# Four hand-written instruction orders changed in an attention, feed-forward and experts kernel on one core

## The chip, the cores and the metric

The kernel runs on one core of a Trainium2 chip. The core has a matrix engine (TensorE, "PE" in the profile, with its weight loads apart as "PEld"), VectorE ("DVE"), ScalarE ("ACT"), GpSimd ("POOL") and the queue that starts most transfers (SyncE, "SP"). Each engine works through its own list of instructions in order; between engines there are only semaphores. The metric is device time of one execution in microseconds (us), the median of some runs. Smaller is better.

## The reference, cut to what matters

Three layers follow one another, all in float32. The kernel computes them in one program.

```python
# 1. attention: q, k, v are (4, 8, 576, 64)
scores = scale * np.matmul(q, k.transpose(0, 1, 3, 2))
kth = np.partition(scores, -32, axis=-1)[..., -32:-31]      # the 32nd largest of each row
scores = np.where(scores >= kth, scores, -1000000000.0)
scores = scores - np.max(scores, axis=-1, keepdims=True)
attn = np.exp(scores)
attn = attn / (np.sum(attn, axis=-1, keepdims=True) + 1e-09)
out = np.matmul(attn, v)                                    # -> x, (2304, 512)
# 2. feed-forward, w_in (512, 2048), w_out (2048, 512)
h = x @ w_in
g = np.maximum(h, 0.0) + np.log1p(np.exp(-np.abs(h)))
x = g @ w_out
# 3. eight experts, w1 (8, 512, 1024), w2 (8, 1024, 512)
logits = x @ w_gate
expert_idx = np.argmax(logits, axis=1)
probs = softmax(logits)                                     # over the 8 experts
out[mask_e] = probs[idx, e][:, None] * (np.maximum(x[mask_e] @ w1[e], 0.0) @ w2[e])
```

## The kernel before, in words

**Blocks and steps.** Attention is cut into 72 blocks. A block is two score tiles of 128 rows by 576 keys. The loop `for i in range(-AHEAD, TAIL)` stands once in each engine's program, and step `i` of it works on several blocks at once: the scores of block `i + 1` (`scores`, L565, copied out by ACT in `scores_out`, L873 and L876), the 32 largest values of block `i` on DVE (`maxima` L1139 and `strike` L1145, four rounds of maxima and three of striking out), the mask and the exponentials of block `i - 1` (`cut_off` L884 on ACT, `mask` on POOL, `exponentials` L891 on ACT), and the product with v of block `i - 2` (`normalise` L897, `turn_probs` L579 and L582, `probs_out` L904, `times_v` L604).

**One block's way through the engines.** DVE finds the maxima. POOL turns them into biases (`biases`), ACT and POOL mask, ACT takes exponentials and sums them into `eps`. DVE turns the sum into `rden` (`reciprocals`, L1153 and L1156). ACT multiplies by it (`normalise`). PE then transposes the nine tiles of probabilities into PSUM (`turn_probs`), ACT copies them to `prT` (`probs_out`), and PE multiplies them with v (`times_v`). `turn_probs(i - 2)` stands behind `scores(i + 1)` on PE and waits until ACT has copied those scores; `probs_out(i - 2)` waits for the semaphore `transit_full`, which the last of the nine transposes raises.

**First stage, steps 0 to 9 (`i < MLP_AT`).** There is no feed-forward work yet. ACT and POOL split the feed-forward weights into a high and a low part in the same steps: `split_wo` (L941) with `low_wo` on POOL and a store by SP behind it, and `split_wi` (L947) with `low_wi`. Here DVE runs `reciprocals(n - 1)` at the end of block `n`. It waits there for `exponentials(n - 1)`, and the next block's maxima stand behind it.

**Second stage, steps 10 to 73.** PE adds one unit of the feed-forward layer to each step: `up` (L634 to L636) and `down` (L653 to L655). ACT and POOL compute the activation of the unit (`rectify`, `logarithm`, `h_high`, `softplus`, `h_low`). For blocks above 10, DVE runs `reciprocals(n - 2)` within block `n`, after the first round of striking out; POOL adds up the sum before it (`denominators`, L1502).

**Hand-over.** Behind the last feed-forward units stands an order written out by hand. The tokens of the last two tiles get their logits (`logits`, L676; copied by `logits_out`, L967). DVE picks the expert (`choose`, L1207 to L1215), PE counts the tokens of each expert (`count_late`, L699 and L700), DVE computes places and tables (`lanes`, `in_slots`, `slot_values`, L1375 to L1422), PE gathers the tables (`slots_late`, L706), and POOL fetches tokens by them. The first two expert tiles run between these steps: `turn_xs` (L716), `e_up` (L727 to L729), `e_relu_out` on ACT (L1010) and `relu` on DVE (L1318), one half of the rectified tile each, `turn_h` (L759), `e_h_out` (L1018) and `h_low` (L1331), `e_down` (L727 to L729). Then a loop over all expert tiles follows, which the change leaves as it is.

Of the kernel before, what the change touches and what calls it, by code (L numbers as in the profile page):

```python
# [20 lines left out]
def build(nc, q, k, v, w_in, w_out, w_gate, w1, w2, out):  # L21
# [15 lines left out]
    KE = EF // P  # L37
# [38 lines left out]
    MLP_AT = 2 * PAIRS + 2  # L76
# [29 lines left out]
    def wo_unit(i):  # L106
        return i - 1 if 0 <= i - 1 < UNITS else None
# [11 lines left out]
    with ExitStack() as ctx:  # L119
# [417 lines left out]
        def _(pe):  # L537
# [249 lines left out]
            for i in range(-AHEAD, TAIL):  # L787
                late = is_block(i - 2)
# [25 lines left out]
            for part in range(2):  # L814
# [26 lines left out]
                                 (1, 2): lambda: turn_tokens(LASTG, NT - 1, 4),  # L841
                                 (1, 3): lambda: logits(NT - 2, 3)}, halves=True, parts=(1,))
            logits(NT - 1, 7)
            turn_xs(1, 1)
            turn_h(0)
            e_up(1, rank_first, {(0, 1): count_late})
            e_down(0, 0, rank_first, {KE // 2: lambda: turn_h(1), KE // 2 + 1: slots_late}, halves=True)
            e_down(1, 1, rank_first, {KE - 2: lambda: turn_xs(2, 2)})
            pe.wait_ge(tiles_ready, 1)
            e_up(2)  # L850
# [15 lines left out]
        def _(act):  # L866
# [156 lines left out]
            for i in range(-AHEAD, TAIL):  # L1023
                now, late = is_block(i - 1), is_block(i - 2)
                if i < MLP_AT:
                    if late:
                        normalise(i - 2, 0)
                        normalise(i - 2, 1)
                    if is_block(i - 3):
                        x_out(i - 3)  # L1030
                    if now:
                        for t in cuts(i - 1):
                            cut_off(i - 1, t)
                    scores_out(i + AHEAD)
                    if wo_unit(i) is not None:
                        split_wo(wo_unit(i))
                    if now:
                        exponentials(i - 1, 0)
                        exponentials(i - 1, 1)
                    if late:  # L1040
                        probs_out(i - 2)
                    if wi_unit(i) is not None:
                        split_wi(wi_unit(i))
                    continue
# [60 lines left out]
            logits_out(NT - 2, 3)  # L1105
            logits_out(NT - 1, 7)

            e_relu_out(0)
            xs_out(1)
            gate_exps(1)  # L1110
            e_h_out(0, 0)
            e_relu_out(1)
            e_h_out(1, 1)
# [18 lines left out]
        def _(dve):  # L1132
# [29 lines left out]
            for n in range(BLOCKS):  # L1162
                for r in range(ROUNDS):
                    for t in range(2):
                        if r:
                            strike(n, t, r)
                    if r == 1 and n > MLP_AT:
                        reciprocals(n - 2)
                    for t in range(2):
                        maxima(n, t, r)  # L1170
# [195 lines left out]
            first_w2(0)  # L1366
            first_w2(1)

            relu(0)
            dve.wait_ge(logits_copied, NT)  # L1370
            choose(LAST, 1)
            xs_low(1)
            gates(LAST, 1)
            dve.wait_ge(counts_ready, 2)
            then(nc.vector.tensor_copy(new_count[:].rearrange("p t e -> p (t e)"),  # L1375
                                       psum[:, 7, 2 * E:4 * E]))
# [299 lines left out]
```

## Time and profile before

| what | us |
|---|---|
| median of 3 runs (lowest 1056.98, highest 1057.76) | 1057.62 |
| the profiled execution, its own time | 1057.62 |
| its span in the trace | 1055.4 |
| busy in the span: PE | 992.1 (94%) |
| busy: DVE | 817.1 (77%) |
| busy: ACT | 727.3 (69%) |
| busy: POOL | 711.8 (67%) |

The profiled execution took 1057.62 us, of which the span from the first to the last instruction is 1055.4; 2.2 us lie around it. The shares are averages over stages that differ much. The first stage ends near 109 us, attention with the feed-forward layer near 755 us, the hand-over near 840 us, and the expert tiles take the rest. The clock column of the windows is the share of its full speed (2.4 GHz) that TensorE was granted: 0.50 is 1.2 GHz. An idle time in brackets at a row's end tells how long the engine was idle before that row and who released it. Durations of rows overlap by a little, because an engine starts an instruction while the one before drains; the distance from one row's start to the next row's start is what an instruction costs its engine.

### The profile page before, as it was taken

The page shows a single profiled execution, that of the slowest core. Times are in us where ns is not written, and L with a number is a line of the kernel's source. Part 1 is how long each engine was busy: PE and PEld are TensorE (multiplying, and loading weights), DVE is VectorE, ACT ScalarE, POOL GpSimd, SP SyncE. Part 2 cuts the span into 40 slices and gives each one's busy share as a digit, 9 for nine tenths or more (in the row PEclk, how much of TensorE's full clock was granted, in tenths as well). Part 3 has the DMA queues.
Part 4 walks back from the last instruction along what each step waited for, and adds up shares of the span by engine and source line. Part 5 has one row for each costly group of instructions (what it writes and reads, how often), then busy time and mean ns, then how long its engine had stood idle before and what let it go on. Part 6 is the DMA issues. An engine that isn't in the chain of part 4 may idle for free.

```text
span 1055.4 us, 21464 instructions
## 1 busy us (share of the span) xinstructions
PE 992.1 (94%) x6878; PEld 806.1 (76%) x6879; DVE 817.1 (77%) x1744; ACT 727.3 (69%) x1390; POOL 711.8 (67%) x831
## 2 busy tenths in 40 slices
PE   3467899999999999999999999999999999999996
PEld 1344687788788788788788888888887788888875
DVE  7999999999999999999999999994345622222261
ACT  2888798889999998998988999998555111111140
POOL 2688899889899899899888899898351311111101
PEclk9855899999999999999999999999999999999999
DMA  9723225343335443323444332333481421111100
GB/s 316 252 90 130 102 93 206 126 145 120 110 113 182 140 159 120 115 107 120 157 154 148 123 120 100 121 120 120 143 328 69 165 95 52 40 40 40 40 20 20
DMA packets 43390, 130.98 MB, mean 124 GB/s; under 512 B 4320, under 2 KB 18656, under 8 KB 33056
## 3 DMA queue, kind: packets, MB, share of 16 engines
q1 hardware_dynamic: 40256, 120.09, 32.3%
q0 software_dynamic: 3040, 9.70, 2.7%
q8 instruction: 51, 0.84, 0.3%
q14 instruction: 43, 0.35, 0.1%
HBM read 111.95 MB, written 18.09 MB: 123 GB/s over the span
## 4 chain that ended last, share of the span: by engine, by line
PE 82%; DVE 7%; POOL 3%; ACT 3%; issue 2%; DMA 1%; SPq 1%; ACTq 0%; DVEq 0%; POOLq 0%
PE psum L604 9%; PE psum L565 8%; PE psum L634 7%; PE psum L727 6%; PE psum L729 6%; PE psum L728 6%; PE psum L653 6%; PE psum L636 6%; PE psum L635 6%; PE psum L655 6%; PE psum L654 6%; PE psum L579 5%; DVE top L1139 3%; DVE work L1145 2%; PE psum L759 2%
## 5 line engine op out<-in xcount | busy, mean ns | idle before, releaser
L1139 DVE MAX8 top<-work 128x8 f32<-128x576 f32 x432 | 305.5, 752 | 0.0
L1145 DVE MATCH_REPLACE8 work<-top,work 128x576 f32<-128x576 f32 x288 | 212.7, 750 | 0.0
L634 PE MATMUL psum<-x_parts,wi_hi 128*128 128x256 f32 x576 | 171.1, 297 | 0.0
L635 PE MATMUL psum<-x_parts,wi_hi 128*128 128x256 f32 x576 | 163.0, 283 | 0.0
L636 PE MATMUL psum<-x_parts,wi_lo 128*128 128x256 f32 x576 | 162.9, 283 | 0.0
L1514 POOL TENSOR_SCALAR pr<-sc,top 128x576 f32<-128x576 f32 x64 | 142.5, 2226 | 6.4
L604 PE MATMUL psum<-prT,vtok 128*64 128x128 f32 (+3 forms) x1600 | 117.1, 286 | 13.6 <-ACT prT L904 13.6
L604 PEld LDWEIGHTS psum<-prT,vtok 128*64 128x64 f32 (+1 forms) x1600 | 85.5, 144 | 52.7 <-issue 42.6
L565 PE MATMUL psum<-kT,qT 64*128 64x512 f32 (+3 forms) x640 | 112.8, 479 | 13.5 <-ACT sc L876 8.9
L1619 POOL DMA_INDIRECT out<-ys,dst_now x19 | 19.2, 1012 | 153.9 <-DVE ys L1341 151.9
L1510 POOL TENSOR_TENSOR pr<-sc,pr 128x576 f32<-128x576 f32 x80 | 114.2, 1432 | 9.2 <-ACT pr L884 9.2
L653 PE MATMUL psum<-wo_ring,h_hi 128*128 x288 | 119.1, 414 | 1.0 <-POOL h_lo L1528 0.9
L1522 POOL TENSOR_TENSOR hs<-hs,ab 128x512 f32<-128x512 f32 x72 | 93.6, 1300 | 34.3 <-ACT ab L927 33.9
L634 PEld LDWEIGHTS psum<-x_parts,wi_hi 128*128 128x128 f32 x576 | 109.9, 191 | 6.6 <-issue 2.0
L891 ACT ACTIVATE pr<-pr,bias 128x576 f32<-128x576 f32 x144 | 110.0, 766 | 4.9 <-POOL pr L1510 3.1
L655 PE MATMUL psum<-wo_ring,h_lo 128*128 x288 | 113.1, 393 | 0.0
L654 PE MATMUL psum<-wo_ring,h_hi 128*128 x288 | 112.7, 391 | 0.0
L565 PEld LDWEIGHTS psum<-kT,qT 64*128 64x128 f32 (+1 forms) x640 | 57.4, 195 | 70.0 <-issue 64.4
L635 PEld LDWEIGHTS psum<-x_parts,wi_hi 128*128 128x128 f32 x576 | 110.2, 191 | 0.2
L636 PEld LDWEIGHTS psum<-x_parts,wi_lo 128*128 128x128 f32 x576 | 110.2, 191 | 0.0
L897 ACT ACTIVATE pr<-pr,rden 128x576 f32<-128x576 f32 x144 | 104.4, 784 | 6.4 <-DVE rden L1156 6.4
L1139 DVE MAX8 top<-sc 128x8 f32<-128x576 f32 x144 | 101.6, 751 | 7.7 <-ACT sc L876 7.7
(206 smaller groups left out, 2235.1 us busy)
## 6 DMA issues: line engine op xcount, KB each, us to landing
wo_ring<-wo_parts SPq DMA_DIRECT2D x72, 1024.0 KB, 4.8
wo_parts<-wo_ring SPq DMA_DIRECT2D x8, 1024.0 KB, 3.9
kT<-in_k SPq DMA_DIRECT2D x16, 288.0 KB, 3.6
qT<-in_q SPq DMA_DIRECT2D x16, 288.0 KB, 4.4
vtok<-in_v SPq DMA_DIRECT2D x16, 256.0 KB, 2.8
wo_raw<-in_moe_w_out SPq DMA_DIRECT2D x1, 4096.0 KB, 14.1
wi_raw<-in_moe_w_in SPq DMA_DIRECT2D x4, 1024.0 KB, 14.6
x_rows<-x2tok SPq DMA_DIRECT2D x16, 256.0 KB, 2.5
```

The costliest lines, as they stand in the source:

```text
L565: mm = nc.tensor.matmul(to[rows, :], qT[h * HD:(h + 1) * HD, p, cols], kT[h * HD:(h + 1) * HD, p, keys], start=True, stop=True)
L604: mm = nc.tensor.matmul(x_raw_at[h * HD:(h + 1) * HD, cols], vtok[rows, p, c, h * HD:(h + 1) * HD], probs, start=(c == 0), stop=(c == FULL))
L634: nc.tensor.matmul(ps[:, part, :], wi_hi[:, u, kk, f], hi, start=first, stop=False)
L635: nc.tensor.matmul(ps[:, part, :], wi_hi[:, u, kk, f], lo, start=False, stop=False)
L636: mm = nc.tensor.matmul(ps[:, part, :], wi_lo[:, u, kk, f], hi, start=False, stop=last)
L653: nc.tensor.matmul(psum[:, 6 + a, :], high, hi, start=(f == 0), stop=False)
L654: nc.tensor.matmul(psum[:, 6 + a, :], high, lo, start=False, stop=False)
L655: mm = nc.tensor.matmul(psum[:, 6 + a, :], low, hi, start=False, stop=(f == KF - 1))
L1139: nc.vector.max(top[:, at, 8 * r:8 * r + 8], sc[:, at, :] if r == 0 else work[:, t, :]).then_inc(topk_step, 1)
L1145: nc.vector.match_replace(work[:, t, :], top[:, at, 8 * r - 8:8 * r], sc[:, at, :] if r == 1 else work[:, t, :], TAKEN).then_inc(topk_step, 1)
L1510: nc.gpsimd.tensor_tensor(to, sc[:, at, :], to, ALU.subtract).then_inc(masked, 1)
L1514: nc.gpsimd.tensor_scalar(to, sc[:, at, :], top[:, at, TOPK - 1:TOPK], OUT, ALU.is_lt, ALU.mult).then_inc(mask_step, 1)
```

## The change

No instruction is added or removed. Four orders change.

1. ACT, steps 2 to 9: `probs_out(i - 2)` moves from behind `split_wo` and the two `exponentials` to a place right behind `scores_out(i + 1)`.
2. DVE, second stage: `reciprocals(n - 2)` moves from the round `r == 1` to the round `r == 2` of block `n`, for n above 10.
3. PE, hand-over: `count_late` moves ahead of `turn_xs(1, 1)` and `turn_h(0)`, out of `e_up(1)`. `slots_late` moves from ahead of product 5 of `e_down(0)` to ahead of its product 3, and so ahead of `turn_h(1)`, which stays ahead of product 4.
4. ACT and DVE, hand-over: ACT runs `gate_exps(1)` ahead of `e_relu_out(0)`. DVE runs `choose(LAST, 1)` ahead of `relu(0)` and `gates(LAST, 1)` ahead of `xs_low(1)`.

```diff
             logits(NT - 1, 7)
+            count_late()
             turn_xs(1, 1)
             turn_h(0)
-            e_up(1, rank_first, {(0, 1): count_late})
-            e_down(0, 0, rank_first, {KE // 2: lambda: turn_h(1), KE // 2 + 1: slots_late}, halves=True)
+            e_up(1, rank_first)
+            e_down(0, 0, rank_first, {KE // 2 - 1: slots_late, KE // 2: lambda: turn_h(1)}, halves=True)
...
                     scores_out(i + AHEAD)
+                    if late:
+                        probs_out(i - 2)
                     if wo_unit(i) is not None:
                         split_wo(wo_unit(i))
                     if now:
                         exponentials(i - 1, 0)
                         exponentials(i - 1, 1)
-                    if late:
-                        probs_out(i - 2)
                     if wi_unit(i) is not None:
                         split_wi(wi_unit(i))
...
+            gate_exps(1)
             e_relu_out(0)
             xs_out(1)
-            gate_exps(1)
...
-                    if r == 1 and n > MLP_AT:
+                    if r == 2 and n > MLP_AT:
                         reciprocals(n - 2)
...
-            relu(0)
             dve.wait_ge(logits_copied, NT)
             choose(LAST, 1)
+            relu(0)
+            gates(LAST, 1)
             xs_low(1)
-            gates(LAST, 1)
             dve.wait_ge(counts_ready, 2)
```

**ACT, one step of the first stage.** Before, the score copies are followed by the cast of the second weights, the exponentials, and then the copy to `prT`:

```order
L873 ACTIVATE sc<-psum 128x128
L876 ACTIVATE sc<-psum 128x512 x2
L941 CAST wo_ring<-wo_raw 128x1024
L891 ACTIVATE pr,eps<-pr,bias 128x576 x2
L904 COPY prT<-psum 128x1152
L947 CAST wi_hi<-wi_raw 128x1024
L897 ACTIVATE pr<-pr,rden 128x576 x2
```

The same place in the changed program, where every line number is one higher:

```order
L874 ACTIVATE sc<-psum 128x128
L877 ACTIVATE sc<-psum 128x512 x2
L905 COPY prT<-psum 128x1152
L942 CAST wo_ring<-wo_raw 128x1024
L892 ACTIVATE pr,eps<-pr,bias 128x576 x2
L948 CAST wi_hi<-wi_raw 128x1024
L898 ACTIVATE pr<-pr,rden 128x576 x2
```

The copy out of PSUM now stands ahead of the cast and the exponentials.

**DVE, one block of the second stage.** Before, the reciprocal follows the first striking out:

```order
L1139 MAX top<-sc 128x8 x2
L1145 MATCH_REPLACE work<-top,sc 128x576 x2
L1156 RECIPROCAL rden<-den 128x2
L1139 MAX top<-work 128x8 x2
L1145 MATCH_REPLACE work<-top,work 128x576 x2
```

In the changed program it follows the second:

```order
L1140 MAX top<-sc 128x8 x2
L1146 MATCH_REPLACE work<-top,sc 128x576 x2
L1140 MAX top<-work 128x8 x2
L1146 MATCH_REPLACE work<-top,work 128x576 x2
L1157 RECIPROCAL rden<-den 128x2
```

Two maxima and two strikings now come ahead of the reciprocal that did not.

**PE, the hand-over.** Before, behind the last logits come the transposes of tokens and of `hr`, and the counts stand behind the first products of `e_up(1)`:

```order
L676 MATMUL psum<-wg,x2T 128x8 x4
L716 MATMUL psum<-ident,xs 128x128 x4
L759 MATMUL psum<-ident,hr 128x128 x8
L736 REGISTER_ALU
L727 MATMUL psum<-w_hi,xsT_hi 128x512
L728 MATMUL psum<-wbuf,xsT_hi 128x512
L729 MATMUL psum<-w_hi,xsT_lo 128x512
L699 MATMUL psum<-onehot,tri 128x16
L700 MATMUL psum<-onehot,ones 128x16
```

In the changed program:

```order
L676 MATMUL psum<-wg,x2T 128x8 x4
L699 MATMUL psum<-onehot,tri 128x16
L700 MATMUL psum<-onehot,ones 128x16
L716 MATMUL psum<-ident,xs 128x128 x4
L759 MATMUL psum<-ident,hr 128x128 x8
L736 REGISTER_ALU
L727 MATMUL psum<-w_hi,xsT_hi 128x512
```

The two counting products have moved ahead of twelve transposes.

## Rows read from the trace of the kernel before

**Rows 1.** Windows: start:end, length, busy of PE, PEld, DVE, ACT, POOL, clock, DMA, GB/s.

```profile
60.00:80.00 20.00, 14.38 (x76) 9.68 (x74) 19.93 (x47) 17.61 (x32) 17.20 (x17) 0.50 0.26 105
...
440.00:460.00 20.00, 20.00 (x158) 16.59 (x157) 19.46 (x43) 18.59 (x38) 18.65 (x21) 1.00 0.43 152
```

**Rows 2.** ACT timeline, step 3: start, duration, operation, count, idle before.

```profile
38.60 1.04 ACT L947 CAST wi_hi<-wi_raw 128x1024 fp32r<-128x1024 f32 x1 [2.13 <-DMA wi_raw<-in_moe_w_in]
39.55 1.44 ACT L897 ACTIVATE pr<-pr,rden 128x576 f32<-128x576 f32 x2
...
43.49 1.05 ACT L941 CAST wo_ring<-wo_raw 128x1024 fp32r<-128x1024 f32 x1
...
48.90 0.78 ACT L897 ACTIVATE pr<-pr,rden 128x576 f32<-128x576 f32 x1 [0.88 <-DVE rden L1156]
```

**Rows 3.** ACT timeline, one whole step (step 7) of the first stage.

```profile
78.58 1.44 ACT L897 ACTIVATE pr<-pr,rden 128x576 f32<-128x576 f32 x2 [0.97 <-DVE rden L1156]
...
82.82 1.06 ACT L941 CAST wo_ring<-wo_raw 128x1024 fp32r<-128x1024 f32 x1
83.75 0.80 ACT L891 ACTIVATE pr<-pr,bias 128x576 f32<-128x576 f32 x1
...
85.39 1.12 ACT L904 COPY prT<-psum 128x1152 f32<-128x1152 f32 x1
86.41 1.05 ACT L947 CAST wi_hi<-wi_raw 128x1024 fp32r<-128x1024 f32 x1
88.48 0.78 ACT L897 ACTIVATE pr<-pr,rden 128x576 f32<-128x576 f32 x1 [1.02 <-DVE rden L1156]
```

**Rows 4.** PE timeline, the transposes of probabilities in that step.

```profile
83.20 1.94 PE L579 MATMUL psum<-ident,pr 128*128 128x128 f32 x8 [1.56 <-ACT sc L876]
84.93 0.42 PE L582 MATMUL psum<-ident,pr 128*128 128x128 f32 x1
```

**Rows 5.** DVE timeline, the sum at the end of that step's block.

```profile
88.10 0.14 DVE L1153 TENSOR_REDUCE den<-eps 128x2 f32<-128x4 f32 x1
```

**Rows 6.** PE timeline, the same transposes at the other clock.

```profile
133.92 1.06 PE L579 MATMUL psum<-ident,pr 128*128 128x128 f32 x8
134.82 0.27 PE L582 MATMUL psum<-ident,pr 128*128 128x128 f32 x1
```

**Rows 7.** ACT and PE timelines, step 9, the last of the first stage.

```profile
98.37 1.44 ACT L897 ACTIVATE pr<-pr,rden 128x576 f32<-128x576 f32 x2 [1.03 <-DVE rden L1156]
...
105.68 1.10 ACT L904 COPY prT<-psum 128x1152 f32<-128x1152 f32 x1
...
106.83 0.48 PE L604 MATMUL psum<-prT,vtok 128*64 128x128 f32 x2 [1.75 <-ACT prT L904]
```

**Rows 8.** Waits of the whole run: who for whom, us in total, times, longest.

```profile
DVE rden L1156 <- POOL den L1502: 24.1, 27, 8.6
...
ACT pr L897 <- DVE rden L1156: 6.4, 7, 1.1
```

**Rows 9.** DVE, ACT and PE timelines, the beginning of the second stage.

```profile
121.64 0.17 DVE L1156 RECIPROCAL rden<-den 128x2 f32<-128x2 f32 x1 [1.00 <-POOL den L1502]
...
124.48 1.41 DVE L1139 MAX8 top<-work 128x8 f32<-128x576 f32 x2
...
150.74 0.17 DVE L1156 RECIPROCAL rden<-den 128x2 f32<-128x2 f32 x1
...
151.69 0.79 ACT L897 ACTIVATE pr<-pr,rden 128x576 f32<-128x576 f32 x1
...
152.84 0.38 PE L579 MATMUL psum<-ident,pr 128*128 128x128 f32 x2
```

**Rows 10.** PE and DVE timelines, the hand-over to the experts.

```profile
809.59 0.33 PE L759 MATMUL psum<-ident,hr 128*128 128x128 f32 x1 [0.27 <-ACT hr L1010]
...
809.89 0.18 DVE L1213 TENSOR_TENSOR onehot<-r_eq,tidx 128x16 f32<-128x16 f32 x1
...
821.11 0.41 PE L759 MATMUL psum<-ident,hr 128*128 128x128 f32 x2 [0.89 <-DVE hr L1318]
```

## The prediction, made before the changed kernel was run

> **What bounds the kernel now.** I read the windows first, because the shares of the page average over unlike stages. They show two regimes [rows 1]. In the first stage DVE is busy 19.93 of 20 us and TensorE 14.38, at a granted clock of 0.50 (its level of 1.2 GHz). In the second stage TensorE is busy 20.00 of 20 at clock 1.00 (2.4 GHz), with DVE at 19.46 close behind. So in the first stage time is lost by whatever makes a block's step longer than DVE's own, and in the second by whatever holds up TensorE.
>
> Then I read one step of the first stage on the ACT timeline [rows 3]. From one multiplication by rden (78.58) to the next (88.48) it is 9.90 us, and ACT waited only 1.02 us of that, for DVE. DVE starts the sum that ACT waits for at 88.10, and its row shows no wait [rows 5]: DVE came straight from its maxima. The page's list of waits says the same: ACT waits for rden 7 times, 6.4 us in all [rows 8]. ACT is nearly as full as DVE here, and its order fits closely: while PE transposes from 83.20 to 84.93 + 0.42 = 85.35 [rows 4], ACT does the weight cast (82.82) and the exponentials (83.75), and reaches the copy to prT at 85.39, when the transposes have just ended.
>
> **Edit 1, the copy to prT ahead of cast and exponentials.** The copy still needs the end of the transposes, and these still need the score copies. So ACT now stands idle from 82.82 until 85.39, which is 2.57 us, with nothing to do. Behind it in its list are the weight cast (POOL's low part and SP's store wait for it), the exponentials (DVE's sum and its next block wait for them) and the next multiplication. The new step on ACT, from rows: from the multiplication to the end of the score copies 43.49 - 39.55 = 3.94 [rows 2], wait 2.57, copy to prT 86.41 - 85.39 = 1.02, cast 83.75 - 82.82 = 0.93, exponentials 85.39 - 83.75 = 1.64 [rows 3], second cast 39.55 - 38.60 = 0.95 [rows 2]. The sum is 11.05 us against 9.90, so 1.15 us more per step, and ACT takes DVE's place as the bound.
>
> How many steps: steps 4 to 8 are whole, 5 x 1.15 = 5.75. In step 2 ACT waited 2.13 us for the load of the weights [rows 2], and the new wait falls almost wholly into that; I take 0.2. Step 3 had its transposes at the higher clock, where nine of them take 134.82 + 0.27 - 133.92 = 1.17 [rows 6] instead of 2.15. The wait is then about 1.6 and the step 3.94 + 1.6 + 4.54 = 10.1, against 48.90 - 39.55 = 9.35 [rows 2]: 0.75. Step 9 therefore begins 0.2 + 0.75 + 5.75 = 6.7 us late. In step 9 the copy to prT came 105.68 - 98.37 = 7.31 us after the multiplication, held by exponentials that wait for masks [rows 7]. Now it goes ahead of them: 3.94, less about 0.7 because this step cuts off one tile and not two (an estimate: half of the 1.44 that a pair of this shape takes in [rows 3]), plus 2.57, is 5.8. That gives 1.5 back. The product with v that opens the dense work of TensorE (106.83 [rows 7]) starts 6.7 - 1.5 = 5.2 us late, and from there on TensorE has no gaps to make it up. **Term 1: +5.2 us.** Bounds of the wait, which the trace does not show in this place: 1.6 with transposes at clock 1.00 and 2.57 at 0.50. I take the second, since [rows 1] has the whole stage at 0.50.
>
> A rule speaks against this term. The Trainium skill, "Perfetto Trace Analysis", section "Identifying the Most-Contended Engine", ranks engines by occupancy, though for TensorE it prefers other measures. Read over the whole span it would leave a stall on ACT (69% busy) unpriced, and the time would stay at 1057.6. The trace disagrees for this stage: there DVE has 19.93 of 20 and ACT 17.61.
>
> **Edit 2, the reciprocal one round later.** It moves past one round of maxima and striking. From the reciprocal at 121.64 to the next round of maxima at 124.48 it is 2.84 us [rows 9], of which such a round takes some 2.78 and the reciprocal the rest (an estimate). Waiting behind the reciprocal are ACT's multiplication and PE's transposes. In the middle of the stage this is covered. There DVE waits for POOL's sum again and again (27 waits, 24.1 us, of which 8.6 and 2.9 come after its last block [rows 8]), so DVE will run up to 2.78 us ahead, and the reciprocal again comes right after the sum. At the beginning it isn't covered, since DVE arrives late from the first stage. Step 8 now begins at 88.48 + 0.2 + 0.75 + 4 x 1.15 = 94.03, and its exponentials end 3.94 + 2.57 + 1.02 + 0.93 + 1.64 = 10.10 later, at 104.13. DVE's sum follows at 104.2 instead of 88.10 + 9.90 = 98.0 [rows 3, 5], so DVE is 6.2 us late. In step 14 the reciprocal stood at 150.74 [rows 9]. It moves by 6.2, by 2.78 for the round, and by -1.09 for the wait before 121.64 that goes with its restart [rows 9]: 7.9. With 0.2 to release ACT it allows the multiplication at 158.84. Without edit 2 that would be at 151.69 + 5.2 = 156.89 [rows 9]. The transposes need the first half of it, 0.92 later, so 159.76, against 152.84 + 5.2 = 158.04 [rows 9]. **Term 2: +1.7 us.** A DVE block takes (150.74 - 121.64) / 3 = 9.70 us here [rows 9], and TensorE's steps are longer on the mean, or DVE would not wait 25 times. So some steps later the lag is gone, but TensorE keeps what it lost. Bounds: 0, if ACT's slack before the transposes is larger than it looks, and 2.8, the whole round.
>
> **Edits 3 and 4, the hand-over.** The choice of experts is ready at 809.89 + 0.18 = 810.07 [rows 10]. The counts now stand ahead of the transposes of hr on PE, and both halves of hr are now made after DVE's choice and ACT's gate exponentials. So these transposes move from 809.59 to about 811.0, 1.4 us later. The tokens' low parts wait behind DVE's five gate operations (about 0.2 us each, an estimate by the 0.18 of [rows 10]), and e_up(1) starts some 1.5 us late, less the counts that have left it. But what ends last is DVE's chain from the counts to the tables. It began behind gates and low parts before and does so now, at the same time. PE waited for it 0.89 us before the transposes at 821.11 [rows 10]. PE now comes later and waits less, and slots_late fills the place of the 0.89. Bounds: -0.9 (that wait gone and nothing added) and +1.6 (nothing absorbed). I take 0, since the chain on DVE is as long as before. The tables come a little earlier for POOL's gathers, which nobody waits for. **Term 3: 0.**
>
> **Sum.** 5.2 + 1.7 + 0 = +6.9 us on a span of 1055.4, so 1062.3. The profiled execution had 2.2 us around its span and took 1057.62, which is also the median of the runs. Forecast: **1064.5 us**.
>
> **The rivals.**
> *The clock decides for less.* If TensorE is granted 1.00 through the first stage, the wait is 1.6 and a step 10.1, only 0.2 above 9.90. Step 9 begins 0.2 + 0.75 + 1.0 = 2.0 late and gives back 2.4, so PE is at -0.4. DVE is at +1.5, and the late reciprocal then costs 2.6. Sum +2.2: 1059.8. For it: step 3 had the higher clock. Against: TensorE has even less to do per us than in [rows 1]. The Trainium skill, "TensorE: Matmul & The Clock Gate", section "What's actually happening", says that activity releases the throttle. By that rule a thinner stage stays at 0.50, and the trace agrees so far as its busy stretch has 1.00 and its thin one 0.50.
> *Nothing is lost.* The transposes' end is modelled. If their semaphore came well before 85.35, ACT would wait little, and its 1.02 us of slack would take it. Then 1057.6. Against: the same transposes at the other clock take 1.17 [rows 6], about half of the 2.15, so the model follows the clock.
> *Faster.* DVE's 12.6 us of waits inside the second stage (24.1 - 8.6 - 2.9) [rows 8] are what edit 2 frees. If DVE, and not TensorE, paced that stage, they would come back: 5.2 - 12.6 = -7.4, so 1050.2. It decides from the point at which ACT's multiplications there are released by DVE. Against: the 7 waits of ACT for rden [rows 8] are those of the first stage, as at 48.90, 78.58, 88.48 and 98.37 [rows 2, 3, 7], and TensorE shows 20.00 of 20 [rows 1].
> *Worse.* The late reciprocal also delays ACT's exponentials, POOL's sum and so the next reciprocal. If this ring can't run at 9.7 us, the lag of term 2 grows by a few tenths per step through the seven steps until 200 us: +3 more, 1067.5.
>
> **How the numbers follow.** Chances: forecast 0.70 (its own range, with both bounds of terms 2 and 3 at once, is +4.3 to +9.6, so 1061.9 to 1067.2), clock 0.12, nothing lost 0.06, faster 0.05, worse 0.07. A difference under 0.2%, 2.1 us, can't be told from none, so "same" is 1055.5 to 1059.7. The clock case lies at that edge and is shared out: faster 0.05, same 0.10, slower 0.85. The range reaches from the clock case to the worse case: 1059.5 to 1067.5.
>
> **What would show it.** Term 1: in steps 4 to 8, ACT's copy to prT is idle before for about 2.5 us with TensorE as releaser, DVE's sum waits for ACT by about 1 us, a step takes 11.05, and the clock stays 0.50 past 113 us. Term 2: ACT's multiplications of steps 11 to 16 wait for rden, by up to 2 us, and none after 210 us; the waits of DVE for the sum shrink. Term 3: a wait of about 1.4 us before the counts, none at the second transposes of hr, and the expert loop entered at the old time plus 6.9. I am wrong if steps 4 to 8 keep 9.9 us, or if TensorE shows waits inside the second stage that take back its lag.

## The result and the profile after

| | before | after |
|---|---|---|
| median of the runs | 1057.62 us (5 runs, 1056.98 to 1058.06) | 1065.46 us (5 runs, 1063.24 to 1068.03) |
| profiled execution | 1057.62 us, span 1055.4 | 1067.26 us, span 1065.0 |

The medians differ by 7.8 us, where +6.9 (1064.5) was forecast. The ratio, which takes in four more runs of the changed kernel, is 1.0078, with a 95% interval of 1.0063 to 1.0092, or +6.7 to +9.7 us. The changed kernel also scatters more: its five runs lie within 4.8 us, where the kernel before has 1.1 here and 1.5 to 2.0 in the larger batches below. Its profiled execution lies at the slow end, so the trace below shows more loss (+9.6) than the median has.

Where the loss arises is read from the starts of a few instructions that both kernels have. The table gives, in us, the place in before, and how much later it is in the profiled execution of each kernel. T(n) are TensorE's transposes of block n; the column before the last is the third turn of hr, after which the experts' loop runs at the old pace.

| profiled execution | product with v that opens the dense work | T(8) | T(9) | T(10) | T(71) | third turn of hr | whole |
|---|---|---|---|---|---|---|---|
| before | 106.83 | 115.79 | 124.28 | 133.92 | 738.21 | 839.94 | 1057.62 |
| after | +3.98 | +3.23 | +5.87 | +8.52 | +8.47 | +9.61 | +9.64 |
| edit 1 alone | +2.35 | +1.54 | +1.55 | +1.50 | +2.17 | +2.31 | +2.36 |
| edit 2 alone | -0.10 | -1.29 | +0.03 | +0.10 | +0.90 | +1.05 | +1.12 |
| edits 3, 4 alone | +0.31 | -0.32 | -0.31 | -0.33 | -0.35 | +0.09 | +0.15 |
| edits 2, 3, 4 | -0.38 | -1.13 | -0.23 | -0.17 | +0.63 | +1.89 | +1.93 |

Three places carry the loss of the changed kernel: the first stage, the step from block 8 to block 10, and the hand-over. Its lag does not grow in the 600 us between T(10) and T(71).

Small differences in the first columns are no effects. The kernel before and those with edit 2 alone, edit 3 alone, edits 3 and 4 (with and without fill) and edits 2, 3 and 4 have the same instructions up to there. Their product with v lies between 106.45 and 107.24 and their T(8) between 114.50 and 115.79, and before, from which all lags are counted, has the latest T(8) of the six.

**The first stage.** One step of ACT in the changed kernel, the answer to [rows 3] (line numbers are one higher now):

```profile
83.01 1.44 ACT L898 ACTIVATE pr<-pr,rden 128x576 f32<-128x576 f32 x2
...
89.51 1.12 ACT L905 COPY prT<-psum 128x1152 f32<-128x1152 f32 x1 [2.44 <-PE psum L582]
90.53 1.05 ACT L942 CAST wo_ring<-wo_raw 128x1024 fp32r<-128x1024 f32 x1
91.47 0.78 ACT L892 ACTIVATE pr<-pr,bias 128x576 f32<-128x576 f32 x1
...
93.00 1.03 ACT L948 CAST wi_hi<-wi_raw 128x1024 fp32r<-128x1024 f32 x1
93.94 1.44 ACT L898 ACTIVATE pr<-pr,rden 128x576 f32<-128x576 f32 x2
```

The copy to prT waits 2.44 us for the transposes and everything else of the step stands behind it. From one multiplication to the next it is 93.94 - 83.01 = 10.93 us, where [rows 3] have 9.90. DVE's sum, which had no wait in [rows 5], now has one:

```profile
93.13 0.16 DVE L1154 TENSOR_REDUCE den<-eps 128x2 f32<-128x4 f32 x1 [0.93 <-ACT pr L892]
```

The step before this one is shorter, 83.01 - 72.94 = 10.07:

```profile
72.94 1.44 ACT L898 ACTIVATE pr<-pr,rden 128x576 f32<-128x576 f32 x2
...
78.58 1.12 ACT L905 COPY prT<-psum 128x1152 f32<-128x1152 f32 x1 [1.58 <-PE psum L582]
```

The same copy waited 1.58 us only. The windows say why: start and end, length, busy time of PE, PEld, DVE, ACT and POOL, then the clock. (The clock column needs care at the start of a trace. In before it shows 1.00 up to about 44 us, though the eight transposes at 33.07 take 1.97 us, as at clock 0.50. Below, only later windows are used, and the transposes' durations beside them: 1.94 us for eight at 0.50, 1.06 at 1.00.)

```profile
60.00:80.00 20.00, 12.39 (x68) 7.97 (x66) 18.06 (x42) 15.97 (x30) 15.74 (x16) 0.59 0.26 105
44.50:75.00 30.50, 21.20 (x111) 14.51 (x111) 27.59 (x63) 23.45 (x41) 23.76 (x23) 0.50 0.21 87
75.20:78.40 3.20, 1.14 (x9) 0.97 (x9) 3.20 (x8) 1.80 (x5) 3.03 (x4) 0.96 0.32 131
78.60:95.50 16.90, 11.88 (x65) 7.82 (x65) 15.82 (x37) 14.46 (x26) 13.91 (x13) 0.51 0.20 81
```

In the stretch of [rows 1] DVE fell from 19.93 to 18.06 of 20 us and TensorE from 14.38 to 12.39. The clock isn't 0.50 all through the stage, it goes up to 1.00 for short stretches, and transposes that fall into one are over in about half the time: at 77.26 eight of them take 1.08 us, in the next step, at 87.32, 1.94.

**Blocks 8 to 10.** The page's list of waits, the answer to [rows 8] (who for whom: us, times, longest):

```profile
DVE rden L1157 <- POOL den L1503: 26.8, 27, 8.6
...
ACT prT L905 <- PE psum L582: 18.2, 9, 2.4
...
DVE den L1154 <- ACT pr L892: 6.4, 7, 2.0
...
ACT pr L898 <- DVE rden L1157: 2.9, 2, 2.5
```

The copy to prT is new in the list with 18.2 us in 9 waits. ACT's waits for the reciprocal went from 7 to 2, and one of them has 2.51 of the 2.9 us. It is here, in ACT's, DVE's and TensorE's own rows, where [rows 9] had no such wait:

```profile
128.37 0.75 DVE L1146 MATCH_REPLACE8 work<-top,work 128x576 f32<-128x576 f32 x1
129.03 0.16 DVE L1157 RECIPROCAL rden<-den 128x2 f32<-128x2 f32 x1
```

```profile
129.23 1.44 ACT L898 ACTIVATE pr<-pr,rden 128x576 f32<-128x576 f32 x2 [2.51 <-DVE rden L1157]
```

```profile
130.15 1.73 PE L579 MATMUL psum<-ident,pr 128*128 128x128 f32 x7 [2.82 <-ACT pr L898]
```

The reciprocal of block 9 comes at 129.03, behind the striking of the round it was moved past. ACT's multiplication had waited 2.51 us for it and TensorE's transposes 2.82 us for ACT. Then come these windows:

```profile
123.00:129.60 6.60, 4.32 (x34) 3.58 (x32) 6.60 (x15) 4.09 (x11) 6.04 (x9) 0.98 0.00 0
129.80:136.50 6.70, 6.35 (x20) 5.46 (x21) 6.70 (x15) 5.96 (x12) 4.06 (x5) 0.52 0.00 0
```

Behind the wait TensorE has the clock 0.50 for a whole stretch of dense work, 6.35 of 6.7 us busy. By 136.7 it is at 1.00 again. In before the clock is 1.00 without a break from 113.3 to 1050 us. From T(9) to T(10) it is 12.29 us against 9.64, so this stretch cost 2.65 us more. It is a loss of this execution. That every run of the changed kernel has it isn't shown, and the medians leave little room for it: edit 1 alone (+4.6) and edits 2, 3 and 4 (+2.7) already add to 7.3 of the 7.8 us.

**The hand-over**, the answer to [rows 10]:

```profile
818.65 0.44 PE L699 MATMUL psum<-onehot,tri 128*128 128x16 f32 x2 [1.29 <-DVE onehot L1214]
818.92 0.59 PE L700 MATMUL psum<-onehot,ones 128*128 128x16 f32 x2
819.35 1.09 PE L716 MATMUL psum<-ident,xs 128*128 128x128 f32 x4
820.24 1.92 PE L759 MATMUL psum<-ident,hr 128*128 128x128 f32 x8
```

```profile
819.30:822.50 3.20, 3.04 (x14) 2.67 (x15) 1.71 (x10) 1.60 (x4) 0.00 (x0) 0.53 0.01 3
```

The counts wait 1.29 us for DVE's choice, and behind this wait too the clock is 0.50 for over 3 us, so that the 8 transposes of hr take 1.92 us instead of the 1.04 that they take in the experiments below at clock 1.00.

What holds TensorE at the end of the hand-over is DVE's chain from the counts to the tables. In before it starts at 812.30, as soon as the counts are there:

```profile
812.30 0.17 DVE L1375 COPY new_count<-psum 128x16 f32<-128x16 f32 x1 [0.62 <-PE psum L700]
```

In the changed kernel the counts come early, but the tokens' low part ahead of the chain waits for ACT's `xsT_hi`, which waits for the transposes of tokens, and these stand behind the counts now:

```profile
821.52 0.69 DVE L1324 TENSOR_TENSOR xsT_lo<-psum,xsT_hi 128x512 fp32r<-128x512 f32 x1 [1.32 <-ACT xsT_hi L1004]
822.13 0.17 DVE L1376 COPY new_count<-psum 128x16 f32<-128x16 f32 x1
```

The choice is 8.53 us later than before (818.42 against 809.89), the start of the chain 9.83. So the chain starts 1.30 us late, and it ends as late: `lanehot` is written at 829.66 instead of 819.84, and TensorE's tables (L706) start at 830.13, at the moment it is done.

### The profile page after: what moved, and what is told of

Read it like the earlier page. It is cut to its first block, busy times and chain, and to the rows that moved or that the text cites. A ratio compares the mean times of both kernels' runs of the same rounds, so it can differ in the third digit from the quotient of the medians.

```text
span 1065.0 us, 21464 instructions
## 1 busy us (share of the span) xinstructions
PE 994.3 (93%) x6878; PEld 809.2 (76%) x6879; DVE 817.9 (77%) x1744; ACT 726.6 (68%) x1390; POOL 712.0 (67%) x831
## 4 chain that ended last, share of the span: by engine, by line
PE 83%; ACT 6%; DVE 3%; issue 3%; POOL 2%; DMA 1%; SPq 1%; ACTq 0%; DVEq 0%; POOLq 0%
PE psum L604 8%; PE psum L565 7%; PE psum L634 7%; PE psum L579 7%; PE psum L727 6%; PE psum L729 6%; PE psum L728 6%; PE psum L653 6%; PE psum L636 6%; PE psum L635 6%; PE psum L655 6%; PE psum L654 6%; PE psum L759 2%; PE psum L676 1%; DMA wo_raw<-in_moe_w_out 1%
## 5 line engine op out<-in xcount | busy, mean ns | idle before, releaser
L579 PE MATMUL psum<-ident,pr 128*128 128x128 f32 x576 | 83.0, 289 | 32.8 <-ACT sc L877 28.9
```

The source lines that it names most:

```text
L579: mm = nc.tensor.transpose(transit[:, j // 3, j % 3 * P:(j % 3 + 1) * P], pr_of(n)[:, first_key(t) + c * P:first_key(t) + (c + 1) * P], id ...
```

## The experiments

Twelve kernels, each timed beside the kernel before on the same chip. Differences below are of medians of one batch; the interval is that of the ratio, which need not be the ratio of the medians. One unit in the third decimal of a ratio is 1.06 us.

| kernel | median | before | ratio, 95% interval |
|---|---|---|---|
| edit 1 alone | 1062.02 | 1057.42 | 1.0041 (1.0027 to 1.0054) |
| edit 2 alone | 1058.76 | 1057.42 | 1.0013 (1.0004 to 1.0022) |
| edits 3 and 4 alone | 1058.40 | 1057.42 | 1.0010 (1.0001 to 1.0019) |
| edits 2, 3 and 4 | 1060.07 | 1057.42 | 1.0027 (1.0016 to 1.0038) |
| copy between cast and exponentials | 1056.75 | 1057.48 | 0.9993 (0.9984 to 1.0002) |
| copy early in step 9 alone | 1056.72 | 1057.48 | 0.9996 (0.9987 to 1.0005) |
| after, first six reciprocals as before | 1064.52 | 1057.48 | 1.0062 (1.0048 to 1.0076) |
| after, filled first stage | 1063.69 | 1057.48 | 1.0056 (1.0042 to 1.0070) |
| edits 3 and 4, filled wait | 1057.86 | 1057.63 | 1.0003 (0.9994 to 1.0012) |
| edit 3 alone | 1058.21 | 1057.63 | 1.0006 (0.9997 to 1.0015) |
| before, filled first stage | 1056.74 | 1057.63 | 0.9992 (0.9983 to 1.0001) |
| copy between in steps 2 to 8, early in 9 | 1057.06 | 1057.63 | 0.9995 (0.9986 to 1.0004) |

### The edits one by one

**Edit 1 alone.**

```diff
+                    if late:
+                        probs_out(i - 2)
                     if wo_unit(i) is not None:
...
-                    if late:
-                        probs_out(i - 2)
```

> The kernel before with edit 1 alone: the copy to prT ahead of cast and exponentials in the first stage. Theory A (ACT's wait for the transposes costs time in every step there): the copy waits about 2.5 us in steps 4 to 8, the product with v that opens the dense work starts 4 to 5 us late (106.83 before), and TensorE keeps that to the end without losing more at the start of the second stage, because the reciprocal still stands behind the first round. So +4 to +5: 1062. Rival B (the time is lost by the late reciprocal and the hand-over, and the first stage only shifts waits about): within 1.5 us of the kernel before.

Measured: +4.6 us by the medians. Theory A holds, rival B falls. In its trace the product with v comes 2.35 us late (theory A had 4 to 5), ACT's copy waits as in the changed kernel, and the transposes of block 9 have only the short wait:

```profile
87.78 1.12 ACT L904 COPY prT<-psum 128x1152 f32<-128x1152 f32 x1 [2.45 <-PE psum L582]
```

```profile
125.83 0.63 PE L579 MATMUL psum<-ident,pr 128*128 128x128 f32 x4 [0.20 <-ACT pr L897]
```

Its five runs lie between 1059.98 and 1062.76, the profiled one being the lowest. In its step 5 eight transposes take 1.17 us and the step 10.16, in its step 7 they take 1.94 and the step 10.93, which shows what a run can win. Steps 4 to 6 are all of the short kind (10.20, 10.16 and 10.08).

**Edit 2 alone.**

```diff
-                    if r == 1 and n > MLP_AT:
+                    if r == 2 and n > MLP_AT:
```

> The kernel before with edit 2 alone: the reciprocal one round later. Theory A: DVE isn't late from the first stage, so the 2.78 us of a round, less the 1.09 us wait that goes, leave the reciprocals of the first blocks of the second stage about 1.7 us later, and ACT's slack takes most of it: 0 to +1, so 1058. Rival B: the late reciprocal costs by itself what the changed kernel lost at the start of the second stage, +2.8 or more (1060.5 and above). Rival C: DVE's waits of 12.6 us inside the stage come back as time, below 1055.

Measured: +1.3 us, between A and B. Rival C falls: DVE's waits for POOL's sum are 25.3 us in 25 times, where before has 24.1 in 27, and no time came back. ACT's multiplications of four blocks wait:

```profile
123.39 1.44 ACT L897 ACTIVATE pr<-pr,rden 128x576 f32<-128x576 f32 x2 [1.20 <-DVE rden L1156]
...
133.09 1.44 ACT L897 ACTIVATE pr<-pr,rden 128x576 f32<-128x576 f32 x2 [0.76 <-DVE rden L1156]
...
152.50 0.78 ACT L897 ACTIVATE pr<-pr,rden 128x576 f32<-128x576 f32 x1 [0.76 <-DVE rden L1156]
```

These steps are 9.70 us apart, which is DVE's block, where TensorE alone needs 9.46. From T(9) to T(13) TensorE loses 0.07, 0.24, 0.24 and 0.20 us, and none from T(13) to T(14). That POOL's sum, and not DVE's place in its list, holds the reciprocal again from there is an inference. In this execution T(8) happened to be 1.29 us early, and the wait of 1.51 us at T(9) took that back: here DVE sets T(9).

**Edits 3 and 4 alone.** The diff is that of the change for these two.

> The kernel before with edits 3 and 4 alone, the hand-over to the experts. Theory A (from the changed kernel's trace, where the lag grew from 8.5 to 9.6 us over the hand-over): about +1.1, half of it a wait of TensorE before the counts and half a stretch at clock 0.50 behind it: 1058.7. Rival B (the prediction's own term 3): 0, the wait of 0.89 us that goes pays for it.

Measured: +1.0 us. In its profiled execution, which was a quick one (1057.77), the wait for the choice is there but the clock stays 1.00:

```profile
809.79 0.40 PE L699 MATMUL psum<-onehot,tri 128*128 128x16 f32 x2 [1.29 <-DVE onehot L1214]
...
810.73 1.04 PE L759 MATMUL psum<-ident,hr 128*128 128x128 f32 x8
...
820.57 2.22 PE L706 MATMUL psum<-inslot,lanehot 128*128 128x108 f32 x18
```

```profile
808.00:823.00 15.00, 12.70 (x74) 10.65 (x74) 12.64 (x46) 3.03 (x7) 0.00 (x0) 1.00 0.01 2
```

DVE's chain is late here too, by less:

```profile
811.97 0.69 DVE L1324 TENSOR_TENSOR xsT_lo<-psum,xsT_hi 128x512 fp32r<-128x512 f32 x1 [0.63 <-ACT xsT_hi L1004]
812.58 0.16 DVE L1376 COPY new_count<-psum 128x16 f32<-128x16 f32 x1
```

The choice is 0.33 us earlier than in before and the chain 0.28 later, so it starts 0.61 us late. From T(71) to the third turn of hr TensorE loses 0.44 us here, against 1.14 in the changed kernel and 1.26 in the kernel with edits 2, 3 and 4, which both have the stretch at 0.50 and a chain that starts 1.30 late. Its runs form two groups: seven from 1057.19 to 1058.42 and three from 1060.02 to 1060.40. One more took 3296 us, an outlier that no median feels. The stretch at 0.50 costs some 0.7 us in those two traces (1.14 against 0.44), less than the 2.4 us between the groups. But it can be longer. The changed kernel with a filled first stage, described below, has the same hand-over; there it lasts twice as long, and the hand-over loses 2.19 us:

```profile
816.60:823.40 6.80, 6.37 (x23) 5.47 (x24) 4.75 (x24) 2.46 (x5) 0.00 (x0) 0.52 0.00 1
```

That such a stretch makes the group at 1060 fits, but no execution of it was profiled.

**Edits 2, 3 and 4.**

> The changed kernel with edit 1 undone, so edits 2, 3 and 4. Theory A: the sum of edit 2 alone (0 to +1) and the hand-over (+1.1), so 1058.7 to 1059.7, and no wait of TensorE of 2.8 us at the transposes of block 9, since DVE isn't late. Rival B (edit 2 costs the same whatever the first stage does): +1.1 and +4, 1062.5 or more.

Measured: +2.7 us (1060.07, 0.4 above theory A's range), where edit 2 alone (1.3) and the hand-over (1.0) add to 2.3. So edit 2 costs about 1.5 us where DVE comes in time, and rival B falls. The wait at block 9 is 1.07 us, and the clock stays 1.00 behind it. With edit 1 alone (4.6) this makes 7.3 us of the 7.8. Whether the rest is an interaction can't be told from differences that are each uncertain by about 1 us.

### How much of the wait must be filled

**The copy between cast and exponentials** (the kernel before, with a half of edit 1).

```diff
                     if wo_unit(i) is not None:
                         split_wo(wo_unit(i))
+                    if late:
+                        probs_out(i - 2)
                     if now:
...
-                    if late:
-                        probs_out(i - 2)
```

> The kernel before with a half of edit 1: the copy to prT stands behind the weight cast and ahead of the exponentials. Theory A (a step costs what ACT's idle wait adds beyond its 1.02 us of slack): the cast fills 0.93 of the wait, so the copy waits about 1.6 us, the step is 10.1 at clock 0.50 (+0.2), step 9 begins 1 to 2 us late and gives 1.5 back: total -0.5 to +0.7, near 1057.5. Rival B (what costs is that the exponentials come behind the copy, and so DVE's sum, whatever ACT's wait): +3 or more.

Measured: -0.7 us, just below theory A's range and, by the interval, no sure gain. The copy waits still, but the cast has taken 0.93 of it, and a step is 10.0 (69.66 - 59.67 = 9.99):

```profile
59.67 1.44 ACT L897 ACTIVATE pr<-pr,rden 128x576 f32<-128x576 f32 x2
...
63.61 1.05 ACT L941 CAST wo_ring<-wo_raw 128x1024 fp32r<-128x1024 f32 x1
66.18 1.12 ACT L904 COPY prT<-psum 128x1152 f32<-128x1152 f32 x1 [1.51 <-PE psum L582]
...
69.66 1.44 ACT L897 ACTIVATE pr<-pr,rden 128x576 f32<-128x576 f32 x2
```

A wait of 1.51 us costs 0.09 us per step, one of 2.44 costs 1.03: it is the part beyond ACT's slack that counts. The slack is not the 1.02 us of [rows 3] alone. ACT's work in a step is 11.05 - 2.57 = 8.48 us by the prediction's own rows, so that of the 9.90 it has 1.42 to spare. A part of the rest is a second wait in the step of [rows 3], for the scores:

```profile
81.69 0.28 ACT L873 ACTIVATE sc<-psum 128x128 f32<-128x128 f32 x1 [0.18 <-PE psum L565]
```

With 8.48 both steps come out: 8.48 + 1.51 = 9.99 and 8.48 + 2.44 = 10.92. Rival B falls, since the exponentials stand behind the copy here too.

**The copy early in step 9 alone.**

```diff
+                    if late and i == MLP_AT - 1:
+                        probs_out(i - 2)
                     if wo_unit(i) is not None:
```

> The kernel before with edit 1 in step 9 alone, the last of the first stage, where the exponentials wait for masks. Theory A: no step is longer, and the product with v comes 1.5 us earlier (105.3 instead of 106.83); TensorE keeps this through the second stage: -1 to -1.5, 1056.2. Rival B: block 9's reciprocal (121.64) or DVE holds TensorE there, and the gain is waited off: 0.

Measured: -0.8 us (-0.4 by the ratio), short of theory A's range and by the interval no sure gain. The product with v comes 1.22 us earlier, at 105.61, and T(71) is 1.02 earlier:

```profile
105.61 0.91 PE L604 MATMUL psum<-prT,vtok 128*64 128x128 f32 x6 [1.21 <-ACT prT L904]
```

In this trace the gain that the prediction gave to step 9 (1.5 us) is there, with 1.22: the product is 0.84 us earlier than in any of the six executions with the old first stage.

**Both places at once.** The copy between cast and exponentials in steps 2 to 8, ahead of both in step 9.

> The kernel before with the copy to prT between the cast and the exponentials in steps 2 to 8, and ahead of both in step 9; nothing else. Theory A: each of the two alone gave -0.7 to -0.8 because step 9's copy comes earlier, and that gain is one and the same: -0.5 to -1.5, 1056.5. Rival B (the gains add): -1.5 or more, 1056.0 or less.

Measured: -0.6 us, as theory A has it; -1.5, where rival B begins, lies at the edge of the interval. No kernel here is surely faster than before.

### The late reciprocal and the clock

**After, with the first six late reciprocals in their old place.**

```diff
-                    if r == 2 and n > MLP_AT:
+                    if r == (1 if n < MLP_AT + 7 else 2) and n > MLP_AT:
```

> The changed kernel with the reciprocals of the first six blocks of the second stage back in their old place, all later ones a round later. Theory A (edit 2 costs only at the start of that stage, where DVE is late, and is covered by POOL's sum in the rest): no wait of TensorE before the transposes of block 9 and no clock of 0.50 behind it, so edit 1 alone (+4.4) and the hand-over (+1.0): 1062.8, against 1065.5 of the changed kernel. Rival B (the late reciprocals cost a little in every block): within 1 us of the changed kernel.

Measured: +7.0 us, 1.7 more than theory A gave and 0.8 less than the changed kernel, so the medians decide nothing. The trace does: the opening product is 5.62 us late, T(9) 5.54 and T(10) 5.49, with no wait for the reciprocal and the clock at 1.00. The loss between blocks 8 and 10 is gone. But the first reciprocal that is late makes ACT wait at block 15, and TensorE is 0.65 us later from there:

```profile
188.37 0.78 ACT L898 ACTIVATE pr<-pr,rden 128x576 f32<-128x576 f32 x1 [1.08 <-DVE rden L1157]
```

So theory A was too narrow: here a late reciprocal costs something at block 15 too. The reading is that DVE hadn't yet got ahead of TensorE there; no run tests it. From there to T(71) the lag stays, 6.14 at T(16) and 6.25.

**After, with the first stage of TensorE filled.** In the two waits of each step TensorE transposes the identity, 9 and 4 times.

```diff
+                if late and i < MLP_AT:
+                    filler(9)
                 if late:
                     turn_probs(i - 2)
+                if late and i < MLP_AT:
+                    filler(4)
```

> The changed kernel with 9 and 4 more transposes of the identity per step in the first stage, in the places where TensorE waits, into a bank that nobody reads there. Theory A (ACT waits for the transposes' duration, and this hangs on the clock): if the fuller stage is granted 1.00, the wait falls from 2.5 to 1.6 us, a step to 10.1, and the time by 3 us or more, to 1062 or less. Rival B (the clock has no part in it): no difference to the changed kernel, or slower by the work added.

Measured: +6.2 us, 1.6 less than the changed kernel and about half of what theory A gave; the two intervals overlap. The mean clock of the stage rose from 0.57 to 0.84, not to 1.00:

```profile
57.00:105.00 48.00, 31.27 (x175) 20.86 (x175) 44.39 (x99) 38.86 (x68) 39.24 (x36) 0.57 0.21 88
```

```profile
57.00:105.00 48.00, 31.78 (x244) 24.18 (x242) 45.02 (x101) 39.68 (x69) 39.42 (x36) 0.84 0.22 88
```

The other executions of this first stage without the fill, edit 1 alone and the one with six reciprocals back, have 0.62 and 0.61. But the transposes that ACT waits for gained nothing: in steps 3 to 9 four of seven still take 1.94 us, as in the changed kernel, and ACT's copies of these steps wait 14.9 us in all, against 15.2 there, 13.8 with edit 1 alone and 16.8 with the six reciprocals back. The product with v is 3.89 us late, against 3.98. So this trace, the slowest of its five runs, does not show the mechanism of theory A; whether the fill saves time stays open. Behind a wait of 3.16 us at block 9 the clock fell here too, as in the changed kernel.

**Before, with the same fill** (6 and 4).

> The kernel before with 6 and 4 more transposes of the identity per step in the first stage, in TensorE's waits. Theory A (DVE bounds that stage, so a higher clock of TensorE is worth nothing there): more of the stage at clock 1.00, steps still 9.90, 1057 to 1057.5. Rival B (the first stage of the kernel before also loses time by the clock): 1056 or less.

Measured: -0.9 us, between the two, and by the interval no sure gain. The steps stay 9.90 us with the mean clock of 57 to 105 us at 0.82 instead of 0.50, as theory A has it: there DVE is the bound. T(8) comes 0.75 us earlier, with clock 0.84 instead of 0.63 in the opening of the dense work, 105 to 116 us. But unfilled executions of the same first stage have T(8) up to 1.29 us earlier, so this isn't shown to be the fill's doing.

**Edits 3 and 4 with the wait filled**, 10 transposes of the identity ahead of the counts.

```diff
+            for _ in range(10):
+                nc.tensor.transpose(psum[:, 4, 0:P], ident[:], ident[:])
             count_late()
```

> Edits 3 and 4 alone, as before, with 10 transposes of the identity ahead of the late counts, where TensorE waits 1.3 us, into a bank that nobody reads there. Theory A (the hand-over costs nothing by its waits, and what it costs comes from executions in which the wait is followed by a stretch at clock 0.50): 1057.5, no loss, and no execution near 1060. Rival B (the delayed transposes of hr cost by themselves): 1058.4 as without the fill, or more.

Measured: +0.2 us, and none of 11 runs above 1058.86, where three of the ten (without the outlier) were at 1060 without the fill. That none is near 1060 fits theory A, but three in ten against none in eleven is thin. Against it, the trace with the wait filled loses the same 0.44 us in the hand-over, and DVE's chain again starts 0.61 us late: the wait before the counts is filled (no idle is left before them), so it isn't that wait which costs the 0.44. Rival B's +0.8 lies within the interval.

**Edit 3 alone.**

> The kernel before with edit 3 alone, the counts and the late slots earlier on TensorE, with the order of DVE and ACT as it was. Theory A: the wait before the counts is the same 1.3 us (it is for DVE's choice), so it has the whole cost of the hand-over: 1058 to 1058.5. Rival B (the later relu and gates of edit 4 carry it): 1057.5.

Measured: +0.6 us, one run of 11 at 1060.33. The wait before the counts is the same 1.29. The hand-over loses 1.11 us in the trace, more than edits 3 and 4 together, and at the same clock of 1.00. The late slots now wait:

```profile
820.67 2.22 PE L706 MATMUL psum<-inslot,lanehot 128*128 128x108 f32 x18 [0.79 <-DVE lanehot L1242]
```

They wait for DVE's chain, which starts 1.25 us late here (at 812.67, with the choice at 809.01): DVE waits 1.79 us for `xsT_hi` and does the five gate operations after it. With edit 4 the gate operations fill that wait, and the chain is 0.61 late. So edit 4 pays for a part of edit 3. In six of the seven traces with edit 3 the loss of the hand-over follows the chain: 0.61 late and 0.44 to 0.46 lost three times, 1.25 to 1.30 late and 1.11 to 1.26 lost three times. The seventh is the one with the long stretch at 0.50: its chain is 1.48 late, and TensorE, itself behind, loses 2.19.

## Why the prediction was right

The time and the main mechanism came out as forecast; the sizes of the steps within term 1, the way in which term 2 arose and the reason given for term 3 did not.

- **Bound of the first stage and edit 1's wait: right.** Forecast 2.57 us idle and a step of 11.05; measured 2.44 and 10.93. The step with transposes at clock 1.00, forecast as 10.1, was 10.07. The half edit confirms that ACT's slack stands between cost and none. The slack is 1.42 us, as the prediction's sum of 11.05 implies, and not the 1.02 that its text names.
- **Term 1, +5.2: near by the medians, for partly wrong reasons.** Edit 1 alone measured +4.6 (interval +2.9 to +5.7), and the product with v was 2.35, 3.98 and 5.62 us late in three traces of the same code. In the changed kernel's trace steps 4 to 8 cost 3.95 us where 5.75 were forecast, because two of the five took 10.07 and 10.56: the reading of [rows 1], a window of 20 us, as a clock of 0.50 for the whole stage was wrong. Step 3 cost 1.58 instead of 0.75. The prediction took its fast transposes for a property of the step, but in the changed kernel they take 1.94. Step 9 gave back 2.15 instead of 1.5. The stage began 0.44 late for no cause that is known. So the rival "the clock decides for less" was half true: not a rival but a part of every execution.
- **Term 2, +1.7: near for edit 2 alone (+1.3), too small in the changed kernel's trace.** DVE's part was forecast well: its reciprocal of block 9 moved by 7.4 us, where 7.9 was worked out. (That sum took 1.09 us for the wait before 121.64, where its row says 1.00.) But the prediction read the loss off step 14 and spread it over steps 11 to 16. It fell at once on block 9, in step 11, since TensorE was only 3.23 us late there and DVE 5.7. As DVE sets T(9), the terms 1 and 2 aren't independent: the less the first stage costs, the longer the wait. At T(9) both together made 5.87, against 6.9. The wait was 2.51, near the upper bound of 2.8, and raised TensorE's lag from 3.23 to 5.87. The step of the argument that failed was to take the wait as the only cost: in this execution the clock of 0.50 behind it cost 2.65 more, which the prediction put at nothing. The announced sign that the waits of DVE for the sum shrink did not come (26.8 us in 27 waits after, 24.1 before).
- **Term 3, 0: too small.** The wait before the counts is 1.29 (forecast 1.4), the one of 0.89 is gone, and DVE's chain does end last, as forecast. What failed is that it begins "at the same time": it begins 0.61 us late at clock 1.00 and 1.30 late at 0.50, because the tokens' low part ahead of it waits for transposes that the counts pushed back. So the tables come later and not, as the prediction has it, a little earlier. Edits 3 and 4 cost +1.0 by the medians, 0.44 in a trace without the low clock, 1.14 and 1.26 in two with it and 2.19 in one with a longer stretch of it.
- **The sum.** +6.9 forecast, +7.8 measured. By the medians term 1 was 0.6 too large and terms 2 and 3 together 1.0 too small (2.7 against 1.7); in the changed kernel's trace it is 1.2 and 3.9. So the agreement of the total owes something to errors of both signs, that is, to luck.
- **The other rivals.** "Nothing is lost" falls by the 18.2 us of ACT's waits, "faster" by edit 2 alone. "Worse", the ring of the late reciprocal, was there in small: 0.07 to 0.24 us in each of four steps of edit 2 alone.

## What to carry to other kernels

Before a copy is moved ahead of filler in an in-order engine's list, take the gap that the filler covered, subtract the engine's slack per step (the step less all of the engine's work in it, not only the one wait that a row shows), and multiply by the steps. Here the slack was 1.42 us: the half edit, with 1.51 us of wait, cost 0.09 us per step, the whole one, with 2.44, 1.03. Where an edit makes TensorE wait, look at its clock behind the wait: a wait of 2.82 us was followed in one execution here by a stretch at half speed that cost 2.65 us more. Where one product is moved ahead, follow what it pushes back: the counts came earlier and the chain that uses them later. Test edits alone: a total that comes out right can hide terms that don't.

## What the hardware did that was not expected

- **The granted clock of the first stage differs between executions of the same instructions.** The kernel with edits 3 and 4 alone has the first stage of before, unchanged. Before shows 0.50 without a break from 55 to 113 us, and its eight transposes at 63.43 take 1.94 us. In the other kernel they start at 63.43 too and take 1.07, and it has 1.00 in three short stretches between 61 and 85 us:

```profile
61.30:64.30 3.00, 0.87 (x8) 0.90 (x9) 3.00 (x7) 3.00 (x7) 2.84 (x3) 1.00 0.58 235
71.50:74.60 3.10, 1.26 (x11) 0.96 (x9) 3.10 (x8) 3.10 (x7) 3.02 (x4) 1.00 0.48 193
81.80:84.80 3.00, 1.18 (x9) 0.97 (x9) 3.00 (x7) 3.00 (x8) 2.92 (x5) 1.00 0.34 137
```

- **The clock can fall in dense work behind a short wait.** It fell behind 2.82 us at 130.15 and behind 1.29 us at 818.65 in the changed kernel, behind 3.16 us in the filled one and behind the 1.29 us of the hand-over in that one and with edits 2, 3 and 4. It did not fall behind the same 1.29 with edits 3 and 4, with edit 3 alone or with the six reciprocals back, or of 1.51 with edit 2 alone. The Trainium skill, "TensorE: Matmul & The Clock Gate", section "What's actually happening", says that activity releases the throttle. The filled first stages agree, with mean clocks of 0.84 where it was 0.57 and 0.82 where it was 0.50. The same section says of a kernel's start that the point of the release varies from run to run; the two executions of one first stage above differ in the middle of a stage as well. Which short waits cost the clock and which don't, no run here settles.
